# Routing and experts of a two-layer MoE block interleaved, with expert weights split ahead of time into a scratch in HBM

## The chip, the cores and the metric

The kernel runs on one core of one Trainium2 chip. The metric is device time in microseconds (us), from start to end of one execution. Everything is fp32 data; most matmuls are done as three products of a rounded "hi" part and a remaining "lo" part, so that the result keeps more than the precision of one product.

Five engines work in parallel, each on its own in-order stream, and meet by semaphores: PE (TensorE, matmuls), DVE (VectorE), ACT (ScalarE), POOL (GpSimd) and SP (SyncE, which here only issues DMAs). DMAs can be issued by SP, ACT and POOL.

## The reference

```python
# 1. gated linear attention, B=4, H=8, S=768, D=48
for t in range(S):
    state = f[:, :, t, :, None] * state + outer(k[t], v[t])
    y[t] = q[t] @ state
x = y as (3072 tokens, 384)
# 2. an MLP
h = x @ w_in                     # 384 -> 2048
x = maximum(0.01 * h, h) @ w_out # 2048 -> 384
# 3. a mixture of 8 experts, each with exactly 3072 / 8 = 384 tokens
logits = x @ w_gate
for idx in argsort(-logits.flatten()):       # greedy over all (token, expert) pairs
    tok, e = idx // 8, idx % 8
    if assigned[tok] < 0 and counts[e] < 384:
        assigned[tok] = e; counts[e] += 1
for e in range(8):
    out[assigned == e] = maximum(x[assigned == e] @ w1[e], 0) @ w2[e]   # 384 -> 1024 -> 384
```

## The kernel before

**Attention and MLP.** The four batches are pipelined: `both(eng, body)` runs `body(None, 0)` (attention of batch 0 alone), three rounds of `body(i, i + 1)` (MLP of batch i beside attention of batch i + 1), and `body(3, None)` (MLP alone). Every engine walks the same list, `schedule(mlp, att)`: 32 slots, each with one `up` (nine matmuls of 128x384 into `ps_h`) and one `down` (nine into `ps_acc`, for the `up` of three slots earlier, `LAG = 3`), and from slot 4 on one step of attention. Between `up` and `down` ACT scales (`leak`, L674), DVE takes the maximum (`leaky`, L836), ACT rounds (`round_g`, L683) and DVE forms the rest (`g_rest`, L843). There are two `ps_h` banks: the `up` of slot j needs the `leaky` of slot j - 2.

SP issues the loads of q, k, f and v for each pair of heads (`load_gates`, L377, and `load`, L391 and L396). It issues nothing else in this stage, so it stands well ahead of the other engines and waits there only for a buffer to come free.

**Routing.** The greedy assignment is done in seven phases, a loop on PE and DVE. A phase finds, for every token, its best open expert (`choose`), then in five rounds narrows down the value at which the first expert fills up: DVE compares 24 tiles of tokens with 32 thresholds (`compare`, L907), PE counts by 24 small matmuls (L1215), DVE and PE pick the interval (L970, L1219, L977). Then the tokens above it are taken, and the full expert is closed. Only when all seven phases and the last step are done does DVE turn the assignment into one list of token numbers, `perm`.

**Experts.** Then `expert_turns` runs experts 0 to 7 in order. Each is 24 + 24 units of three 128x384 matmuls. SP loads the raw weights of the next expert in four pieces of 768 KB (L415), ACT rounds them to `w_hi` (L726), POOL subtracts to get `w_lo` (L522). POOL gathers the expert's tokens by an indirect DMA (L529), PE turns them (`turn_rows`, L1250), and POOL scatters the results to `out` (L541).

Of the kernel before, what the change touches and what calls it, by code (L numbers as in the profile page):

```python
# [30 lines left out]
P = 128  # L31
# [26 lines left out]
PHASE_LINKS = 18  # L58


def gated_attention_two_mlps(nc, qkf, v, w_in, w_out, w_gate, w1, w2, out):
    x2_rows = nc.dram_tensor("x2_rows", (TOKENS, DM), F32, kind="Internal").ap()

    ctx = ExitStack()
    with ctx:
# [7 lines left out]
        w_hi = sb("w_hi", [P, 2, FF * KT], F32R)  # L73
        w_lo = sb("w_lo", [P, 2, FF * KT], F32R)
        w_raw = sb("w_raw", [P, 2, WCH])
        qk = sb("qk", [P, 2, 3, SEQ])
# [21 lines left out]
        x2_out = spare[:, KT * BLK:KT * BLK + ST * DM].rearrange("p (s d) -> p s d", s=ST)  # L98
        gate_w = sb("gate_w", [P, KT, EXPERTS])
# [9 lines left out]
        def carver(whole):  # L109
# [3 lines left out]
            def carve(*shape, dt=F32):  # L113
                n = int(np.prod(shape)) * (2 if dt == BF16 else 4) // 4
                got = whole[:, at[0]:at[0] + n]
# [13 lines left out]
        column = carve(P, dt=BF16)  # L129
        prefer = carve(EXPERTS, TT)  # L130
        slot0 = carve(EXPERTS, TT)
        tile_start = carve(TT)
        row = carve(1)
        earlier = carve(P, dt=BF16)
        ones = carve(P, dt=BF16)
        minus_earlier = carve(P, dt=BF16)
        minus_ones = carve(P, dt=BF16)

        carve = carver(xT[:].rearrange("p k t -> p (k t)"))
        magnitude, chosen, upto = (carve(EXPERTS, TT) for _ in range(3))  # L140

        prefer_open, taken, sure, above_low, maybe, fits = (carve(EXPERTS, TT, dt=BF16) for _ in range(6))
# [7 lines left out]
        open_, penalty = carve(EXPERTS), carve(EXPERTS)  # L150
        slot, slot_row, slot_tile = carve(TT), carve(TT), carve(TT)
        slot_int, slot_bits, slot_tile_bits = (carve(TT, dt=I32) for _ in range(3))

        carve = carver(log_f[:])
        above = carve(TT, WAYS, dt=BF16)
        counted = carve(EXPERTS, TT, dt=BF16)
        row_sure, row_maybe, filled, is_full = (carve(EXPERTS, dt=BF16) for _ in range(4))
        flag = carve(2, dt=BF16)
        restart_tile = carve(EXPERTS, TT, dt=BF16)
        carve = carver(y_pair[:].rearrange("p b n -> p (b n)"))  # L160
        row_hot = carve(TT, P, dt=BF16)
        carve = carver(qk[:].rearrange("p b a n -> p (b a n)"))
        tile_hot = carve(TT, TT, dt=BF16)
        tile_hot_start = carve(TT, TT, dt=BF16)
        tile_hot_row = carve(TT, TT, dt=BF16)
# [57 lines left out]
        y_rows_free = sem("y_rows_free")  # L223
        x2_stored = [sem(f"x2_stored{i}") for i in range(ST)]

        route_consts = sem("route_consts")
        most_local = sem("most_local")
        most_ready = sem("most_ready")
        routed = sem("routed")
        best_ready = sem("best_ready")  # L230
# [4 lines left out]
        keyed_ready = sem("keyed_ready")  # L235
        chosen_ready = sem("chosen_ready")
        sure_ready = sem("sure_ready")
        above_low_ready = sem("above_low_ready")
        penalized = sem("penalized")
        open_ready = sem("open_ready")  # L240
        row_sums_ready = sem("row_sums_ready")
        row_bases_done = sem("row_bases_done")
        slot_row_ready = sem("slot_row_ready")
        tile_hot_ready = sem("tile_hot_ready")
        hot_ready = sem("hot_ready")
        perm_done = sem("perm_done")
        perm_ready = sem("perm_ready")
        ewraw_in = [sem(f"ewraw_in{i}") for i in range(2)]
        ew_hi_done = sem("ew_hi_done")
        ew_lo_done = sem("ew_lo_done")  # L250
# [7 lines left out]
        edown_done = sem("edown_done")  # L258
        y_rows_ready = sem("y_rows_ready")
# [78 lines left out]
        def weight_piece(n, half):  # L338

            if half == 0:  # L340
                return (lambda w: w[:, 0, :].rearrange("p (k f) -> p k f", k=KT)[:, :, n * 512:(n + 1) * 512],
                        w_in.rearrange("(k p) f -> p k f", p=P)[:, :, n * 512:(n + 1) * 512], KT)
# [11 lines left out]
        def expert_turns(eng, turn):  # L354


            with eng.Fori(0, EXPERTS // 2 - 1) as i:
                for q in range(2):
                    turn(i * 2 + q, q, True, i)
# [958 lines left out]
```

## Time and profile before

| what | value |
|---|---|
| three runs | 1054.19, 1056.42, 1056.67 us; median 1056.42 |
| the profiled execution: span, first to last instruction | 1052.9 us |
| its PE, DVE, ACT, POOL busy | 843.3, 516.1, 352.8, 228.9 us |
| mean granted TensorE clock | 0.882 of full speed |
| DMA | 70.16 MB |

The whole execution of a run is the span and a few microseconds around it; the median of the runs is 3.5 us above this span. By stages: attention alone from 0 to about 104 us, three rounds of MLP beside attention to about 544, MLP alone to 656, routing to 817, experts to the end. A "busy" share says how long an engine had an instruction in work, not that it could not have done more.

### The profile page before, as it was taken

The page shows a single profiled execution, that of the slowest core. Times are in us where ns is not written, and L with a number is a line of the kernel's source. Part 1 is how long each engine was busy: PE and PEld are TensorE (multiplying, and loading weights), DVE is VectorE, ACT ScalarE, POOL GpSimd, SP SyncE. Part 2 cuts the span into 40 slices and gives each one's busy share as a digit, 9 for nine tenths or more (in the row PEclk, how much of TensorE's full clock was granted, in tenths as well). Part 3 has the DMA queues.
Part 4 walks back from the last instruction along what each step waited for, and adds up shares of the span by engine and source line. Part 5 has one row for each costly group of instructions (what it writes and reads, how often), then busy time and mean ns, then how long its engine had stood idle before and what let it go on. Part 6 is the DMA issues. An engine that isn't in the chain of part 4 may idle for free.

```text
span 1052.9 us, 16482 instructions
## 1 busy us (share of the span) xinstructions
PE 843.3 (80%) x5665; PEld 813.5 (77%) x5665; DVE 516.1 (49%) x1166; ACT 352.8 (34%) x737; POOL 228.9 (22%) x154
## 2 busy tenths in 40 slices
PE   2547999997999998999999998122322699999995
PEld 2446899997999997999999998122212699999994
DVE  7774755543655434656433333787788222222220
ACT  3233645433545334444323322200000244444431
POOL 7930000000000000000010000400000467777741
PEclk9678999998999998999999999555555799999998
DMA  8544223321023321122000000310000245555520
GB/s 214 142 89 93 42 45 58 79 47 36 13 45 65 77 41 36 42 40 37 25 30 1 1 23 23 122 58 0 0 0 1 75 136 164 164 164 164 165 83 23
DMA packets 53082, 70.16 MB, mean 67 GB/s; under 512 B 28752, under 2 KB 37712, under 8 KB 53008
## 3 DMA queue, kind: packets, MB, share of 16 engines
q1 hardware_dynamic: 44432, 44.06, 17.8%
q0 software_dynamic: 6208, 20.45, 5.9%
q10 hardware_dynamic: 2368, 4.72, 2.2%
q8 instruction: 39, 0.64, 0.3%
q14 instruction: 35, 0.29, 0.1%
HBM read 55.06 MB, written 9.44 MB: 61 GB/s over the span
## 4 chain that ended last, share of the span: by engine, by line
PE 72%; DVE 16%; issue 7%; ACT 2%; DMA 1%; POOL 1%; DVEq 0%; ACTq 0%; POOLq 0%
PE ps_h L1148 9%; PE ps_acc L1148 9%; PE ps_h L1150 9%; PE ps_h L1149 9%; PE ps_acc L1149 9%; PE ps_acc L1150 9%; PE ps_s L1100 4%; PE ps_y L1110 4%; PE ps_s L1215 3%; DVE log_f L907 2%; DVE cum L780 2%; PE ps_y L1115 1%; PE ps_k L1084 1%; DVE rel L786 1%; PE ps_h L1183 1%
## 5 line engine op out<-in xcount | busy, mean ns | idle before, releaser
L1148 PE MATMUL ps_h<-x_hi,w_hi 128*128 128x384 f32 x576 | 207.8, 361 | 11.1 <-issue 8.3
L1150 PE MATMUL ps_h<-x_hi,w_lo 128*128 128x384 f32 x576 | 198.2, 344 | 0.0
L1149 PE MATMUL ps_h<-x_lo,w_hi 128*128 128x384 f32 x576 | 198.2, 344 | 0.0
L836 DVE TENSOR_TENSOR g_full<-ps_h,g_full 128x384 f32<-128x384 f32 x128 | 71.3, 557 | 205.3 <-ACT g_full L674 205.1
L470 POOL DMA_DIRECT2D x_rows<-w_raw x24 | 13.1, 545 | 576.5 <-DVE logits L852 574.2
L1148 PE MATMUL ps_acc<-g_hi,w_hi 128*128 128x384 f32 x384 | 131.0, 341 | 0.0
L1149 PE MATMUL ps_acc<-g_lo,w_hi 128*128 128x384 f32 x384 | 130.0, 339 | 0.0
L1150 PE MATMUL ps_acc<-g_hi,w_lo 128*128 128x384 f32 x384 | 129.8, 338 | 0.0
L522 POOL TENSOR_TENSOR w_lo<-w_raw,w_hi 128x1536 fp32r<-128x1536 f32 x32 | 112.0, 3510 | 45.5 <-ACT w_hi L726 38.2
L1148 PEld LDWEIGHTS ps_h<-x_hi,w_hi 128*128 128x128 f32 x576 | 111.1, 193 | 13.4 <-issue 10.2
L674 ACT ACTIVATE g_full<-ps_h 128x384 f32<-128x384 f32 x128 | 62.5, 489 | 169.1 <-PE ps_h L1150 165.5
L1149 PEld LDWEIGHTS ps_h<-x_lo,w_hi 128*128 128x128 f32 x576 | 111.2, 193 | 0.0
L1150 PEld LDWEIGHTS ps_h<-x_hi,w_lo 128*128 128x128 f32 x576 | 110.8, 192 | 0.0
L1051 DVE SCALAR_TENSOR_TENSOR g_lo<-ps_h,g_hi 128x384 fp32r<-128x384 f32 x64 | 35.6, 557 | 124.8 <-ACT g_hi L740 124.8
L1215 PE MATMUL ps_s<-log_f 128*32 128x8 bf16 x840 | 28.9, 176 | 73.3 <-DVE log_f L931 39.0
L1215 PEld LDWEIGHTS ps_s<-log_f 128*32 128x32 bf16 x840 | 25.5, 103 | 76.3 <-DVE log_f L907 76.3
L616 ACT ACTIVATE y_pair<-ps_y 96x128 f32<-96x128 f32 x96 | 26.2, 273 | 161.0 <-PE ps_y L1115 136.7
L1148 PEld LDWEIGHTS ps_acc<-g_hi,w_hi 128*128 128x128 f32 x384 | 72.1, 188 | 0.0
L1149 PEld LDWEIGHTS ps_acc<-g_lo,w_hi 128*128 128x128 f32 x384 | 72.1, 188 | 0.0
L1150 PEld LDWEIGHTS ps_acc<-g_hi,w_lo 128*128 128x128 f32 x384 | 72.0, 188 | 0.0
L843 DVE TENSOR_TENSOR g_lo<-g_full,g_hi 128x384 fp32r<-128x384 f32 x128 | 70.4, 550 | 0.5
L1100 PE MATMUL ps_s<-q_apart,qk 112*128 112x256 f32 x192 | 66.5, 431 | 4.6 <-DVE scores L824 3.4
(165 smaller groups left out, 1484.9 us busy)
## 6 DMA issues: line engine op xcount, KB each, us to landing
w_raw<-w SPq DMA_DIRECT2D x32, 768.0 KB, 4.4
qk<-qkf SPq DMA_DIRECT2D x32, 288.0 KB, 5.3
qk<-qkf SPq DMA_DIRECT2D x32, 144.0 KB, 5.0
vals<-v SPq DMA_DIRECT2D x32, 144.0 KB, 6.7
x_rows<-w_raw POOLq DMA_DIRECT2D x24, 192.0 KB, 2.2
w_raw<-w_in POOLq DMA_DIRECT2D x4, 768.0 KB, 7.1
w_raw<-w_out POOLq DMA_DIRECT2D x4, 768.0 KB, 5.2
xT<-y_pair ACTq DMA_DIRECT2D x8, 192.0 KB, 5.9
```

The source lines that it names most:

```text
L522: nc.gpsimd.tensor_tensor(place(w_lo, q), w_raw[:, n % 2].rearrange("p (k f) -> p k f", k=tiles), place(w_hi, q).bitcast(F32), ALU.subtrac ...
L616: nc.scalar.activation(y_pair[0:2 * HD, hp % 2, c * P:(c + 1) * P], ps_y[0:2 * HD, 0:P], ACT.Copy).then_inc(y_copied, 1)
L674: nc.scalar.activation(g_full[:, j % 2, :], ps_h[j % 2][:, 0:BLK], ACT.Copy, scale=0.01)\
L836: nc.vector.tensor_tensor(g_full[:, j % 2, :], ps_h[j % 2][:, 0:BLK], g_full[:, j % 2, :], ALU.max).then_inc(g_ready, 1)
L843: nc.vector.tensor_tensor(g_lo[:, b, :], g_full[:, j % 2, :], g_hi[:, b, :].bitcast(F32), ALU.subtract).then_inc(g_lo_ready, 1)
L1051: nc.vector.scalar_tensor_tensor(out=g_lo[:, f % GB, :], in0=ps_h[f % 2][:, 0:CAP], scalar=0.0, in1=g_hi[:, f % GB, :].bitcast(F32), op0=A ...
L1100: nc.tensor.matmul(ps_s[:, 0:2 * P], qk[0:HP, hp % 2, 1, chunk], q_apart[:, :, chunk], start=True, stop=True).then_inc(scores_done, 1)
L1110: last = nc.tensor.matmul(y, vals[:, hp % 2, c, h * HD:h * HD + 2 * HD], scores[:, before % 2, h], start=h == 0, stop=c == 0 and h == 1)
L1148: nc.tensor.matmul(to, a_hi, b_hi, start=start, stop=False)
L1149: nc.tensor.matmul(to, a_hi, b_lo, start=False, stop=False)
L1150: last = nc.tensor.matmul(to, a_lo, b_hi, start=False, stop=stop)
L1215: last = nc.tensor.matmul(ps_s[0:WAYS, 0:EXPERTS], above[:, g, :], counted[:, :, g], start=g == 0, stop=g == TT - 1)
```

## The change

1. **Weights of the experts.** In each of the 32 slots of a round with an MLP, one more item, `prep`, stands behind `up`: SP loads a chunk of 128x384 of `w1` or `w2` into `e_raw` (192 KB), ACT rounds it to `e_hi` (`prep_hi`), DVE subtracts (`prep_lo`, in place), and SP stores both to the scratch `ready_weights` in HBM. Four rounds of 32 chunks are all eight experts. There are two `e_raw` buffers, and `store_prep` issues the load of chunk n + 1 behind the two stores of chunk n.
2. **Routing beside experts.** After each phase the expert that has just filled up is picked (`pick`, with its number in `weight_index`), its list of 384 tokens is formed (`place`, `gather_lists`, `list_tokens`), and it runs next. `expert_order()` merges the phases into the units of the experts by a table of gaps: phase 0 and, up to unit 64, the first part of phase 1 stand ahead of the first expert; a phase then takes 47 units and an expert 48.
3. **Fetch.** POOL fetches the split weights of the picked expert by four indirect DMAs (1.5 MB each), two ahead of the gather of the tokens and two behind. ACT's rounding and POOL's subtraction in the expert stage are gone. POOL's `partition_all_reduce` ahead of phase 0 becomes two small matmuls.

```diff
+        ready_weights = [nc.dram_tensor(f"ready_weights{n}", (EXPERTS * P, 2 * WCH), F32, kind="Internal").ap()
+                     for n in range(4)]
...
                     yield "up", h, j
+                    yield "prep", slot
...
+        def route_order():
+            at = 0
+            for p in range(EXPERTS - 1):
+                for gap, step in ((2, "choose"), (5, "count0"), (2, "ways0"), (3, "count1"), (2, "ways1"),
+                                  (3, "count2"), (2, "ways2"), (3, "count3"), (2, "ways3"), (3, "count4"),
+                                  (2, "ways4"), (4, "rank"), (3, "fill"), (3, "base"), (6, "spot"), (2, "spread")):
+                    at += gap
...
+            def store_prep(mb, n, last):
+                b = n % 2
+                _, _, to = prep_piece(mb, n)
+                sp.wait_ge(prep_hi_done, mb * 2 * FT + n + 1)
+                sp.sem_inc(prep_seen, 1)
+                sp.dma_start(to[0], e_hi[:, b, :]).then_inc(prep_hi_stored[b], 16)
+                sp.wait_ge(prep_lo_done, mb * 2 * FT + n + 1)
+                sp.sem_inc(prep_seen, 1)
+                sp.dma_start(to[1], e_raw[:, b, :]).then_inc(prep_lo_stored[b], 16)
+                if 1 <= n < 2 * FT - 1:
+                    prep_landed(mb, n - 1)
+                    load_prep(mb, n + 1)
...
                     elif what == "load":
                         load(ab, *a)
+                    elif what == "prep":
+                        store_prep(mb, a[0], ab is None)
...
+            def prep_hi(mb, n):
+                act.wait_ge(e_raw_in[n % 2], 16 * (mb * FT + n // 2 + 1))
+                nc.scalar.activation(e_hi[:, n % 2, :].bitcast(F32R), e_raw[:, n % 2, :], ACT.Copy)\
+                    .then_inc(prep_hi_done, 1)
...
+            def prep_lo(mb, n):
+                dve.wait_ge(prep_hi_done, mb * 2 * FT + n + 1)
+                nc.vector.tensor_tensor(e_raw[:, n % 2, :].bitcast(F32R), e_raw[:, n % 2, :], e_hi[:, n % 2, :],
+                                        ALU.subtract).then_inc(prep_lo_done, 1)
...
+            def load_expert(e, n):
+                q = e % 2
+                nc.gpsimd.indirect_dma_start(
+                    out=w[:, q, n].rearrange("p h n -> p (h n)").bitcast(F32), out_offset=None,
+                    in_=ready_weights[n][:, :],
+                    in_offset=bass.IndirectOffsetOnAxis(ap=weight_index[:, e:e + 1], axis=0)).then_inc(ew_in[q][n], 16)
```

**SP's stream at the head of a round of MLP beside attention.** Before, the round begins with the loads of f (48x768), of q and k (48x1536) and of v (128x6x48) for the first pair of heads:

```order
L334 ISA
L377 ISA [waits gates_zeroed0,exp_done]
L377 DMA qk<-qkf 48x768
L377 ISA
L377 DMA qk<-qkf 48x768
L265 REGISTER_ALU
L391 REGISTER_ALU [waits y_done,zeroed0]
L391 DMA qk<-qkf 48x1536
```

Now the stores of the split chunk 0 stand ahead of them, and these wait for ACT and DVE of slot 0 of the same round:

```order
L350 ISA
L483 ISA [waits prep_hi_done]
L483 DMA ready_weights<-w_raw 128x384
L486 ISA [waits prep_lo_done]
L486 DMA ready_weights<-e_raw 128x384
L280 ISA
L447 ISA [waits gates_zeroed0,exp_done]
L447 DMA qk<-qkf 48x768
L447 ISA
L447 DMA qk<-qkf 48x768
L280 REGISTER_ALU
L461 REGISTER_ALU [waits y_done,zeroed0]
```

The loads of the first pairs are no longer free to be issued during the round before.

**SP's stream in the slots of such a round** (there was nothing at this place before; `e_raw<-w` is the load of a chunk, `w_raw` holds `e_hi`):

```order
L486 DMA ready_weights<-e_raw 128x384 [waits prep_lo_done]
L470 ISA [waits prep_hi_stored1,prep_lo_stored1]
L470 DMA e_raw<-w 128x384
L481 REGISTER_ALU
L483 DMA ready_weights<-w_raw 128x384 [waits prep_hi_done]
L486 DMA ready_weights<-e_raw 128x384 [waits prep_lo_done]
```

The load of the next chunk is issued behind the store that waits for this chunk's `prep_lo`.

**DVE's stream in an expert beside a phase.** Before, nothing but `g_lo` and `x_lo` stood in an expert. Now the end of `fill`, all of `base` and the start of `spot` (from `pick` to `gather_lists`) stand between the `g_lo` that PE waits for:

```order
L1073 SCALAR_TENSOR_TENSOR qk<-vals,qk 128x24 [waits routed]
L1123 SCALAR_TENSOR_TENSOR g_lo<-ps_h,g_hi 128x384 [waits eg_hi_ready]
L1080 TENSOR_TENSOR qk<-qk,ps_k 128x24 [waits slot_base_done,reach_ready]
L1081 TENSOR_TENSOR qk<-qk 128x24 [waits routed]
L1082 TENSOR_SCALAR qk<-qk 128x24 [waits routed]
L1083 TENSOR_SCALAR qk<-qk 128x24 [waits routed]
L1084 TENSOR_SCALAR qk<-qk 128x24
L1085 TENSOR_TENSOR qk<-vals,qk 128x24x12 [waits routed]
L1087 TENSOR_TENSOR qk<-qk,vals 128x24x12 [waits routed]
L1088 TENSOR_SCALAR qk<-qk,vals 128x24x12 [waits routed]
L1089 TENSOR_TENSOR qk<-vals,qk 128x768
L1123 SCALAR_TENSOR_TENSOR g_lo<-ps_h,g_hi 128x384 [waits eg_hi_ready]
```

Nine operations on the lists stand between one `g_lo` and the next.

## Rows read from the trace of the kernel before

**Rows 1.** The head of the profile's page

```profile
span 1052.9 us, 16482 instructions
```

**Rows 2.** Windows by stage: start:end, length, busy us of each engine, clock, DMA

```profile
core 0: us, PE busy (x) PEld busy (x) DVE busy (x) ACT busy (x) POOL busy (x), PEclk, DMA share, GB/s
60.00:75.00 15.00, 10.18 (x46) 8.82 (x47) 8.45 (x15) 5.07 (x13) 2.62 (x1) 0.65 0.15 34
549.00:645.00 96.00, 96.00 (x555) 95.89 (x555) 33.78 (x69) 29.78 (x67) 3.25 (x12) 1.00 0.02 7
690.00:823.00 133.00, 35.00 (x820) 28.07 (x820) 102.43 (x364) 0.00 (x0) 5.65 (x5) 0.50 0.02 5
827.00:1010.00 183.00, 182.48 (x1047) 181.73 (x1048) 42.24 (x78) 82.38 (x123) 129.56 (x63) 0.99 0.48 151
```

**Rows 3.** Timeline of the MLP alone: start us, us, engine, line, operation

```profile
549.56 0.49 ACT L674 ACTIVATE g_full<-ps_h 128x384 f32<-128x384 f32 x1 [1.53 <-PE ps_h L1150]
550.09 0.56 DVE L836 TENSOR_TENSOR g_full<-ps_h,g_full 128x384 f32<-128x384 f32 x1 [1.46 <-ACT g_full L674]
...
641.58 0.49 ACT L674 ACTIVATE g_full<-ps_h 128x384 f32<-128x384 f32 x1 [2.28 <-PE ps_h L1150]
...
644.76 0.49 ACT L674 ACTIVATE g_full<-ps_h 128x384 f32<-128x384 f32 x1 [2.27 <-PE ps_h L1150]
```

**Rows 4.** Timeline, ACT: first and last slot of the first round beside attention

```profile
104.35 0.49 ACT L674 ACTIVATE g_full<-ps_h 128x384 f32<-128x384 f32 x1 [2.22 <-PE ps_h L1150]
...
235.61 0.49 ACT L674 ACTIVATE g_full<-ps_h 128x384 f32<-128x384 f32 x1 [2.27 <-PE ps_h L1150]
```

**Rows 5.** DMA issues: tiles, issuer, count, KB each, median us to landing

```profile
w_raw<-w SPq DMA_DIRECT2D x32, 768.0 KB, 4.4
...
qk<-qkf SPq DMA_DIRECT2D x32, 144.0 KB, 5.0
...
x_rows<-w_raw POOLq DMA_DIRECT2D x24, 192.0 KB, 2.2
...
gate_w<-w_gate SPq DMA_DIRECT2D x1, 12.0 KB, 1.8
```

**Rows 6.** Timeline, SP: the loads of one pair of heads

```profile
201.31 0.83 SPq L391 DMA_DIRECT2D qk<-qkf  x2
...
204.00 1.26 SPq L377 DMA_DIRECT2D qk<-qkf  x2
```

**Rows 7.** Window over the landing of these loads

```profile
202.00:210.00 8.00, 8.00 (x53) 7.84 (x52) 3.61 (x9) 2.23 (x6) 0.00 (x0) 1.00 1.06 192
```

**Rows 8.** Timeline of routing: its start, one phase, one count on PE

```profile
655.75 0.36 DVE L936 SCALAR_TENSOR_TENSOR xT<-logits 128x192 f32<-128x192 f32 x1
...
664.11 0.62 DVE L914 TENSOR_REDUCE xT<-logits 128x24 f32<-128x192 f32 x1 [0.20 <-DVE xT L950]
...
694.04 0.62 DVE L914 TENSOR_REDUCE xT<-logits 128x24 f32<-128x192 f32 x1 [0.41 <-DVE xT L1008]
...
711.19 0.17 DVE L1004 TENSOR_SCALAR xT<-ps_y 128x8 f32<-128x8 f32 x1
...
712.61 0.62 DVE L914 TENSOR_REDUCE xT<-logits 128x24 f32<-128x192 f32 x1 [0.39 <-DVE xT L1008]
```

**Rows 9.** Timeline, PE: the count of one round of a phase

```profile
717.72 0.82 PE L1215 MATMUL ps_s<-log_f 128*32 128x8 bf16 x24 [0.94 <-DVE log_f L907]
```

**Rows 10.** The chain that ended last: the first expert's start

```profile
820.99 3.04 DMA xT<-x_rows,perm
824.08 0.91 PE ps_s L1250 x3
...
827.52 0.68 PE ps_h L1148
```

**Rows 11.** Timeline, PE: the same turn of rows in two following experts

```profile
840.59 0.49 PE L1250 MATMUL ps_s<-ident,xT 128*128 128x128 f32 x3
...
867.00 0.49 PE L1250 MATMUL ps_s<-ident,xT 128*128 128x128 f32 x3
```

More of the change, by code:

```diff
@@ L258, in gated_attention_two_mlps @@
         edown_done = sem("edown_done")
+        y_rows_free = sem("y_rows_free")
         y_rows_ready = sem("y_rows_ready")
@@ new lines, in take @@
+            def take(p):
+                dve.wait_ge(row_bases_done, p + 1)
+                link(stt(out=fits, in0=upto, scalar=-(CAP + 0.5), in1=by_tile(ps_k[:, 16:24]),
+                         op0=ALU.add, op1=ALU.is_le))
+                link(tt(fits, fits, maybe, ALU.mult))
+                link(tt(taken, fits, sure, ALU.add))
+                whole_sum(filled, taken).then_inc(filled_ready, 1)
+                link(stt(out=logits[:], in0=taken, scalar=HUGE, in1=logits[:], op0=ALU.mult, op1=ALU.add))
@@ L1057, in _ @@
-            for k in range(KT):
-                rows_rest(0, 0, k)
-            expert_turns(dve, turn)
+            for what, *a in expert_order():
+                if what == "route":
+                    step, p, n = a
+                    if step == "choose":
+                        choose(p)
+                    elif step == "count":
+                        flag_full(p, n)
+                    elif step == "ways":
+                        narrow(p, n)
+                    elif step == "rank":
+                        take(p)
+                    elif step in ("fill", "last"):
+                        pick(p)
+                    elif step == "base":
+                        place(p)
+                    elif step == "spot":
+                        gather_lists(p)
+                    elif step == "spread":
+                        list_tokens(p)
+                elif what == "rows_rest":
+                    e, k = a
+                    rows_rest(e, e % 2, k)
+                elif what == "rest":
+                    g_expert_rest(*a)
@@ L1239, in _, with count_above @@
-            last.then_inc(perm_done, 1)
-            def turn_rows(e, q, k, earlier_users):
+            def count_above(p, n):
+                rnd = p * ROUNDS + n
+                if n == 0:
+                    pe.wait_ge(chosen_ready, p + 1)
+                for g in range(TT):
+                    for m, part in enumerate(PARTS):
+                        if g == part.start:
+                            pe.wait_ge(above_ready, rnd * len(PARTS) + m + 1)
+                    last = nc.tensor.matmul(ps_k[0:WAYS, 0:EXPERTS], above[:, g, :], counted[:, :, g],
+                                            start=g == 0, stop=g == TT - 1)
+                last.then_inc(counts_done, 1)
@@ new lines, in fills, with slot_base, token_lists @@
+            def fills(p):
+                pe.wait_ge(filled_ready, p + 1)
+                nc.tensor.matmul(ps_k[:, 24:32], ones, filled, start=True, stop=True).then_inc(fills_done, 1)
+            def slot_base(p):
+                pe.wait_ge(reach_ready, p + 1)
+                nc.tensor.matmul(ps_k[:, 32:33], earlier, reach[:, TT - 1:TT], start=True, stop=True)\
+                    .then_inc(slot_base_done, 1)
+            def token_lists(p):
+                pe.wait_ge(hots_ready, p + 1)
+                for g in range(TT):
+                    last = nc.tensor.matmul(ps_k[0:WIDE, 40:40 + 2 * SPOTS], wide_hot[:, g, :], spots[:, g, :],
+                                            start=g == 0, stop=g == TT - 1)
+                last.then_inc(narrow_done, 1)
```

684 lines of the change are left out of this document (367 added, 317 removed).

## The prediction

> **What bounds the kernel now.** I read the windows by stage first. In the MLP alone PE is busy for 96.00 of 96.00 us, in the experts for 182.48 of 183.00, both at full clock; in routing for 35 of 133 us at the clock's lower level (0.50, 1.2 GHz), while DVE is busy for 102.43 [rows 2]. So PE bounds everything but routing, and routing is a dialogue of DVE and PE in which no large matmul runs. A phase takes 18.57 us (694.04 to 712.61) [rows 8]. Routing and experts together take 397.2 us, from 655.75 [rows 8] to the end of the span at 1052.9 [rows 1]. An expert takes 26.41 us (840.59 to 867.00) [rows 11], 48 units of three matmuls. A slot of the MLP alone takes 3.18 us, and slots 1 to 31 take 95.2 us (549.56 to 644.76) [rows 3]. The 31 intervals of a round beside attention take 131.3 us (104.35 to 235.61) [rows 4], 4.23 each.
>
> **First part: routing beside experts, a gain.** I lay out the new way from 655.75 to the end.
> - *Prelude.* It took 8.4 us (655.75 to 664.11) [rows 8], most of it in waiting for POOL's reduce over partitions. With two small matmuls in its place I count 3.1 us.
> - *To the first expert.* In the steady phase, choose to the full counts takes 17.2 us (694.04 to 711.19) [rows 8]. `pick`, `place` and the lists add about 16 short DVE operations and the one-hots, which I put at 6.5 us: the list of tokens is there at 23.7. The part of phase 1 up to unit 64 (choose, three counts) stands next in PE's order, about 10 us; the gather of the tokens (three issues, then 3.04 us to land [rows 10]) and the first two weight pieces run beside it. From landed rows to the first `ps_h` it is 3.4 us (824.08 to 827.52) [rows 10]. Together 38 us.
> - *An expert beside a phase.* PE: 26.4 us, and six sets of 24 small matmuls (0.82 us a set [rows 9], of which about 0.65 keep PE from the next matmul) with some 25 changes between kinds of matmul, together 5.5 us: about 32. DVE: 18.57 us of a phase [rows 8], 6.1 more of new work, 11 `g_lo` and `x_lo` of 0.56 [rows 3]: 30.9 if none of the dialogue's waits is filled. Neither alone is over 32. But both streams are in a fixed order: `place` and its neighbours keep DVE for 3.5 us where PE has six units (3.2 us), `choose` with the end of the lists for 5 where PE has seven (3.7) and needs `g_lo` twice in between, and each round's compare takes 1.6 for three units of 1.6. I add 4 us of PE waiting. 36 us per expert; the bounds are 32 (no waiting) and 41 (each such place paid in full).
> - *Sum.* 342 units of phases less the 64 ahead are 278, or 5.8 experts at 36; the other 2.2 run at 26.4. The start and end of the stage beyond eight such experts are 225.4 - 211.3 = 14.1 us (from 827.52 [rows 10] to 1052.9). So 3.1 + 38 + 208.8 + 58.1 + 14.1 = 322 us in place of 397: **-75 us**, bounds -52 (41 us per expert) and -98 (32).
> - *The fetch* moves 6.3 MB of split weights and 1.2 MB of rows per expert. The stage now moves 151 GB/s with the DMA engines 0.48 busy [rows 2], so 315 GB/s if they were full: 24 us per expert, under the 36. Two pieces go ahead of the tokens, 10 us and 2 of latency; about 21 units and a dozen small steps lie between `pick` and `turn_rows`, 14 us. That is just hidden, and I cost it at nothing.
>
> **Second part: the preparation of the weights, a loss.** `prep` puts 128 chunks into slots that PE fills. Its ACT and DVE time (0.49 and 0.56 us each [rows 3]) finds room: in the MLP alone DVE is busy for 34 of 96 us. What counts is the loop it closes. The load of chunk n + 1 is issued only behind the store of chunk n's `lo`, and ACT, in order, stands at `prep_hi` of chunk n + 1 until it has landed, with `leak` of the next slot behind it; PE can be two slots ahead of that and then waits. So a slot cannot be shorter than this round trip, C:
> - ACT rounds and DVE starts: 0.53 us (549.56 to 550.09 [rows 3]); DVE subtracts: 0.56;
> - SP issues the `lo` store: 0.42 (half of a pair's 0.83 [rows 6]), with semaphores and address registers about 0.2 more, then issues the load;
> - its landing, L. No row shows a 192 KB load on SP alone. 12 KB took 1.8 us and 768 KB took 4.4; a 192 KB store 2.2 [rows 5]. Between the first two a straight line gives 2.4, and part of the `lo` store just ahead in the queue makes it 2.6. The lower bound is 2.2; the upper is 5.0, the 144 KB load that stood behind others [rows 5]. I take the near rows, 2.6.
>
> C = 0.53 + 0.56 + 0.42 + 0.25 + 2.6 = 4.4 us, 3.9 with the low L, 5.0 if L is 3.2.
> - *MLP alone:* the first two chunks are there ahead; 30 slots go from 3.18 to 4.4: **+37 us** (+22 to +55).
> - *Three rounds beside attention:* at 4.23 us per interval the loop alone costs little. The head costs more. The loads of q, k, f and v for two pairs used to be issued in the round before; now they stand behind the first `prep` stores of this round, and the load of chunk 2 behind them all, on the same queue. One pair's loads keep the DMA engines full from 202 to 210 us, busy share 1.06 [rows 7], after an issue of 4 us that began at 201.31 [rows 6]; less the latency I count 7 us. Two pairs are 14 us from about 3.5 us into the round, then two stores: chunk 2 lands at 19.4 us. After it come 29 intervals at 4.4, and two more pair loads in mid-round delay a chunk by 2.3 us each: 19.4 + 127.6 + 4.6 = 151.6 us in place of 131.3. **+20 us each, +61 in all**. With C at 3.9 and the head at 16 PE binds again behind the head, and a round costs +12; with C at 5.0, +38.
> - *Clock:* during the head PE is idle, and some matmuls behind it will run at the lower level, as all of routing does (0.50 [rows 2]), and take twice as long. I put +5 us on it for three heads, an estimate without a row of its own.
>
> **Sum.** 1052.9 - 75 + 37 + 61 + 5 = 1081 us of span; with the 3.5 us by which the median of the runs is above this span, **1085 us**. The forecast is a kernel slower by some 29 us.
>
> **Rivals.**
> 1. *The loop is hidden: faster.* If the load lands in under about 1.6 us, or the ring takes the load ahead of the queued stores and pair loads, C falls to the slot's 3.18, the last stage costs nothing, and only some 10 us of waiting for f and q remain per head. Then 1056 - 75 + 30 = 1011 us. It decides at C near 3.8 with a head of 9 us. For it: PE keeps two slots in hand. Against it: the one 192 KB row took 2.2 us to land [rows 5], and the sum of the rest is 1.8. A gain also comes if both bounds meet, -98 and +63. Chance 0.24.
> 2. *The experts wait for their fetch.* POOL now issues seven indirect DMAs for an expert, and DVE is at work on the lists beside it. If the tokens land 4 to 6 us late for each of seven experts: +35, 1120 us. For it: the slack is 2 us by my count. Against: the DMA engines are full for only two thirds of an expert. The stage now says little, since DVE is busy in it for only 42 of 183 us [rows 2]. The Trainium skill ("SBUF — State Buffer", Who interferes with whom) says that DVE in its two-port modes locks GpSimd out of the port it writes DMA descriptors through, and that DMAs issued by SP or ACT are immune; it speaks against moving the fetch from SP to POOL. No row here has POOL issuing beside a busy DVE. Chance 0.12.
> 3. *The clock falls in the last stage.* With C at 4.4 PE is busy for 72% of a slot. In the prologue a stretch with PE busy for 10.18 of 15 us had a mean clock of 0.65 [rows 2]. At 0.65 the 18 matmuls take 4.9 us, and a slot with them: +15, and at the full lower level, 5.8, +42; so 1100 to 1127, say 1110. The Trainium skill ("TensorE: Matmul & The Clock Gate", HAM oscillation — how this bites in real kernels) describes the same: bursts of matmuls between waits for a DMA run slow every time. Against it: a wait of 1.2 us is short beside those of the prologue. Chance 0.12.
> 4. *A longer loop.* L at 3.2 us, from 512-byte rows of `w1` and the store ahead: +18 in the last stage, +54 in the rounds: 1150 us. Chance 0.10.
>
> **How the numbers follow.** The forecast has 0.42, with a range of its own from 1060 to 1110. Rivals 2 to 4 make 0.34, all slower, rival 1 0.24. Measurement tells 0.3% (3 us) from no change. Faster: 0.26, of them 0.24 from rival 1; the same: 0.03, from the overlap of the bounds; slower: 0.71. The range for 8 in 10 leaves out the lower part of rival 1 and the upper part of rival 4: 1012 to 1145.
>
> **What the profile after will show.** If I am right: `leak` of the MLP alone comes every 4.4 us in place of 3.18, with ACT's `prep_hi` waiting for the DMA of `e_raw`; the first slots of a round beside attention take 35 us or more to slot 6 in place of 18; the first expert starts some 41 us after the last logits; six experts take about 36 us each and the last two 26.4. The prediction is wrong if the slots keep 3.18 us (then rival 1), if an expert beside a phase takes 31 or 41 us, or if `turn_rows` waits for the gathered rows (rival 2).

## The result, and the profile after

The changed kernel takes 1152.19 us (median of 4 runs, 1151.73 to 1155.2), the kernel before 1055.41: a ratio of 1.0934, 95% interval 1.0903 to 1.0965. It is slower by 97 us; I had said 29, and the range ended at 1145. The profiled execution of after has a span of 1150.3 us. All differences below are between profiled executions unless a median is named.

The page's head and the chain that ended last:

```profile
span 1150.3 us, 18015 instructions
...
PE 34%; DVE 22%; DMA 19%; issue 10%; ACT 6%; SPq 6%; another core or an unknown queue 1%; ACTq 0%; POOL 0%; DVEq 0%
```

DMA has 19% of the chain, nearly all of it loads of `e_raw`. I mark slots by the start of ACT's `leak` (`g_full<-ps_h`), as in [rows 3, 4]. "Beside attention" stands for the rounds in which MLP and attention share the engines. The parts of the span that changed:

| part | before | after | difference | forecast |
|---|---|---|---|---|
| three rounds beside attention, first slot to first slot | 149.0, 149.0, 145.3 | 183.6, 184.6, 177.6 | +102.6 | +61 and +5 |
| MLP alone, slots 0 to 31 | 97.2 | 131.4 | +34.2 | +37 |
| last logits to the end | 397.2 | 359.5 | -38 | -75 |

What is left, the attention ahead of the first slot, differs by less than 2 us.

**MLP alone.** Timeline of after, the steady state; SPq is SP's queue of issues, the bracket names the idle time ahead and its releaser:

```profile
701.56 0.34 SPq L470 DMA_DIRECT2D e_raw<-w  x1
703.93 0.53 ACT L778 ACTIVATE w_raw<-e_raw 128x384 fp32r<-128x384 f32 x1 [2.77 <-DMA e_raw<-w]
704.36 0.47 ACT L764 ACTIVATE g_full<-ps_h 128x384 f32<-128x384 f32 x1
704.49 0.56 DVE L936 TENSOR_TENSOR e_raw<-e_raw,w_raw 128x384 fp32r<-128x384 f32 x1 [2.60 <-ACT w_raw L778]
...
705.13 0.33 SPq L486 DMA_DIRECT2D ready_weights<-e_raw  x1
...
705.65 0.34 SPq L470 DMA_DIRECT2D e_raw<-w  x1
...
708.02 0.53 ACT L778 ACTIVATE w_raw<-e_raw 128x384 fp32r<-128x384 f32 x1 [2.78 <-DMA e_raw<-w]
```

This is the loop of the forecast, row by row: load issued to ACT 2.37, ACT to DVE 0.56, DVE to the store's issue 0.64, store to the next load's issue 0.52. Together 4.09 us a slot (I had 4.4), where TensorE alone needs 3.18 [rows 3].

**The head of a round.** SP's issues in the second round, whose slot 0 is at 286.25, and ACT's rows beside them:

```profile
287.41 0.37 SPq L483 DMA_DIRECT2D ready_weights<-w_raw  x1
288.04 0.36 SPq L486 DMA_DIRECT2D ready_weights<-e_raw  x1
288.76 0.90 SPq L447 DMA_DIRECT2D qk<-qkf  x2
290.01 0.84 SPq L461 DMA_DIRECT2D qk<-qkf  x2
291.03 1.36 SPq L466 DMA_DIRECT2D vals<-v  x2
...
296.96 0.91 SPq L447 DMA_DIRECT2D qk<-qkf  x2
298.22 0.38 SPq L483 DMA_DIRECT2D ready_weights<-w_raw  x1
298.86 1.20 SPq L486 DMA_DIRECT2D ready_weights<-e_raw  x1
300.52 0.99 SPq L470 DMA_DIRECT2D e_raw<-w  x1
```

```profile
306.27 0.52 ACT L778 ACTIVATE w_raw<-e_raw 128x384 fp32r<-128x384 f32 x1 [10.06 <-DMA e_raw<-w]
```

The loads of two pairs, and those of f for a third, stand between the stores of chunk 0 and those of chunk 1, and the load of chunk 2 comes behind all. It is issued 14.3 us into the round, and ACT gets it at 20.0 us (forecast 19.4), after a wait of 10.06.

**The experts.** `turn_rows` of the eight experts (PE L1370) begin at 831.92, 870.22, 911.37, 954.78, 996.71, 1038.31, 1077.39 and 1104.14: 38.3, 41.1, 43.4, 41.9, 41.6, 39.1 us beside a phase and 26.8 without one. Windows over four of the intervals, columns as in [rows 2]:

```profile
911.00:955.00 44.00, 40.82 (x334) 35.13 (x334) 25.75 (x88) 6.67 (x14) 10.06 (x10) 0.85 0.51 197
955.00:997.00 42.00, 37.22 (x311) 31.79 (x310) 26.28 (x90) 6.67 (x14) 9.87 (x10) 0.95 0.45 170
997.00:1038.00 41.00, 37.01 (x306) 31.74 (x304) 25.29 (x86) 6.66 (x14) 9.86 (x10) 0.91 0.54 208
...
1077.00:1104.00 27.00, 26.87 (x157) 26.45 (x156) 6.33 (x12) 6.67 (x14) 9.70 (x10) 1.00 0.80 324
```

The clock is below 1.00 beside phases and 1.00 in the last, which has none. Timeline of PE and windows of 2 us around one first count show when it falls:

```profile
904.57 0.33 PE L1263 MATMUL ps_h<-x_hi,w 128*128 128x384 f32 x1
906.19 0.80 PE L1327 MATMUL ps_k<-qk 128*32 128x8 bf16 x24 [1.29 <-DVE qk L1012]
...
909.17 0.18 PE L1333 MATMUL ps_k<-qk,vals 32*128 32x1 bf16 x1 [0.78 <-DVE qk L1019]
```

```profile
906.00:908.00 2.00, 1.81 (x30) 1.69 (x30) 0.90 (x3) 0.00 (x0) 1.54 (x2) 0.97 0.69 184
908.00:910.00 2.00, 1.22 (x5) 0.82 (x4) 0.74 (x4) 0.00 (x0) 0.00 (x0) 0.50 0.94 356
...
916.00:918.00 2.00, 2.00 (x9) 1.93 (x9) 1.65 (x6) 0.49 (x1) 0.00 (x0) 0.50 0.02 6
918.00:920.00 2.00, 2.00 (x32) 1.71 (x31) 0.50 (x2) 0.00 (x0) 0.00 (x0) 0.97 0.00 0
```

TensorE waits 1.29 us for `choose`, runs 24 small matmuls, and within 2 us the clock is at its lower level for some 10 us. Between 840 and 1104 us it falls five times (at about 884, 908, 949, 966 and 1031 us), each time within 3 us of the end of a wait of 0.8 to 1.6 us, or during one, and stays low for 3 to 10 us. The length of a wait does not tell it alone. After a longer one (DVE's `g_lo` stood behind `choose`; the row names no releaser) the clock stayed at 1.00:

```profile
990.76 0.45 PE L1261 MATMUL ps_h<-x_hi,w 128*128 128x384 f32 x1 [2.13 <-issue]
```

```profile
991.00:993.00 2.00, 2.00 (x31) 1.71 (x31) 0.00 (x0) 0.00 (x0) 0.95 (x1) 1.00 0.74 193
```

### The profile page after: what moved, and what is told of

It is laid out like the page before. It is cut to its first block, busy times and chain, and to the rows that moved or that the text cites. A ratio compares the mean times of both kernels' runs of the same rounds, so it can differ in the third digit from the quotient of the medians.

```text
span 1150.3 us, 18015 instructions
## 1 busy us (share of the span) xinstructions
PE 905.3 (79%) x5828; PEld 836.2 (73%) x5828; DVE 595.8 (52%) x1438; ACT 369.4 (32%) x833; POOL 146.9 (13%) x156
## 4 chain that ended last, share of the span: by engine, by line
PE 34%; DVE 22%; DMA 19%; issue 10%; ACT 6%; SPq 6%; another core or an unknown queue 1%; ACTq 0%; POOL 0%; DVEq 0%
DMA e_raw<-w 19%; PE ps_h L1261 5%; PE ps_acc L1261 4%; PE ps_h L1263 4%; PE ps_h L1262 4%; DVE e_raw L936 4%; PE ps_acc L1262 3%; PE ps_acc L1263 3%; ACT w_raw L778 3%; SPq L486 2%; PE ps_k L1327 2%; PE ps_s L1213 2%; DVE cum L868 2%; PE ps_y L1223 2%
## 5 line engine op out<-in xcount | busy, mean ns | idle before, releaser
L1261 PE MATMUL ps_h<-x_hi,w 128*128 128x384 f32 x576 | 219.6, 381 | 54.2 <-DVE g_full L924 30.9
L1262 PE MATMUL ps_h<-x_lo,w 128*128 128x384 f32 x576 | 202.8, 352 | 0.0
L1263 PE MATMUL ps_h<-x_hi,w 128*128 128x384 f32 x576 | 202.5, 351 | 0.0
L1261 PEld LDWEIGHTS ps_h<-x_hi,w 128*128 128x128 f32 x576 | 114.3, 198 | 68.1 <-DVE g_full L924 33.7
L936 DVE TENSOR_TENSOR e_raw<-e_raw,w_raw 128x384 fp32r<-128x384 f32 x128 | 71.1, 556 | 160.3 <-ACT w_raw L778 160.0
L1261 PE MATMUL ps_acc<-g_hi,w 128*128 128x384 f32 x384 | 135.0, 352 | 9.6 <-ACT w_raw L789 6.0
L1262 PE MATMUL ps_acc<-g_lo,w 128*128 128x384 f32 x384 | 132.9, 346 | 0.0
L1263 PE MATMUL ps_acc<-g_hi,w 128*128 128x384 f32 x384 | 132.3, 345 | 0.0
L1262 PEld LDWEIGHTS ps_h<-x_lo,w 128*128 128x128 f32 x576 | 114.9, 199 | 0.0
L1263 PEld LDWEIGHTS ps_h<-x_hi,w 128*128 128x128 f32 x576 | 114.4, 199 | 0.0
L1261 PEld LDWEIGHTS ps_acc<-g_hi,w 128*128 128x128 f32 x384 | 75.0, 195 | 11.4 <-issue 6.3
L1262 PEld LDWEIGHTS ps_acc<-g_lo,w 128*128 128x128 f32 x384 | 74.8, 195 | 0.0
L1263 PEld LDWEIGHTS ps_acc<-g_hi,w 128*128 128x128 f32 x384 | 74.3, 194 | 0.0
L1261 PE MATMUL ps_acc<-w,g_hi 128*128 128x384 f32 x192 | 74.1, 386 | 0.0
```

Source lines behind the costliest of these rows:

```text
L936: nc.vector.tensor_tensor(e_raw[:, n % 2, :].bitcast(F32R), e_raw[:, n % 2, :], e_hi[:, n % 2, :], ALU.subtract).then_inc(prep_lo_done, 1)
L1261: nc.tensor.matmul(to, a_hi, b_hi, start=start, stop=False)
L1262: nc.tensor.matmul(to, a_hi, b_lo, start=False, stop=False)
L1263: last = nc.tensor.matmul(to, a_lo, b_hi, start=False, stop=stop)
```

## The experiments

The theory: the round trip of a chunk and the order of SP's queue cost the 137 us of the rounds and the MLP alone, and the clock beside phases costs part of the experts' gain. The rivals: the added passes of ACT and DVE, or the added DMA traffic, cost it whatever the order.

**Load first.** `store_prep` waits for the buffer and issues the next load ahead of this chunk's stores:

```diff
             def store_prep(mb, n, last):
+                if 1 <= n < 2 * FT - 1:
+                    prep_landed(mb, n - 1)
+                    load_prep(mb, n + 1)
                 ...
                 sp.dma_start(to[1], e_raw[:, b, :]).then_inc(prep_lo_stored[b], 16)
-                if 1 <= n < 2 * FT - 1:
-                    prep_landed(mb, n - 1)
-                    load_prep(mb, n + 1)
```

> The load of the next chunk, and its waits for the two stores that free its buffer, stand ahead of the waits and stores of this chunk on SP's queue, so a chunk's load no longer hangs behind ScalarE's and VectorE's work on the chunk before. Theory (a slot can't be shorter than the round trip store - landing - load - landing - ScalarE - VectorE): the round trip now spans two slots, the MLP alone goes from 4.2 us a slot back to 3.2 to 3.4 (-27 to -34 us), the three rounds lose some 10 us each (the stall at the head of a round stays): 1080 to 1095 us. Rival (the added passes of ScalarE and VectorE in their in-order streams fill the slot by themselves): MLP alone stays over 4.0 us a slot and the time over 1135. Second rival (DMA traffic itself lengthens the MLP's transfers): the same.

1112.31 us, ratio 1.0554 (1.0500 to 1.0607); MLP alone 120.3 us, rounds 176.8, 175.5, 172.2. It took 11 us off the MLP alone, not 27 to 34, and 5 to 9 off a round; the expected 1080 to 1095 and the rivals' 1135 were both missed. The timeline shows what was left:

```profile
690.49 0.37 SPq L489 DMA_DIRECT2D ready_weights<-e_raw  x1
...
693.33 0.39 SPq L470 DMA_DIRECT2D e_raw<-w  x1
693.83 0.42 SPq L486 DMA_DIRECT2D ready_weights<-w_raw  x1
694.36 0.37 SPq L489 DMA_DIRECT2D ready_weights<-e_raw  x1
...
697.16 0.39 SPq L470 DMA_DIRECT2D e_raw<-w  x1
```

From one low store to the landing that SP waits for is 2.8 us, and the next load and the next two stores stand behind that wait: 3.9 us from store to store (690.49 to 694.36). The loop had only moved into SP's own queue.

**Chunks issued by GpSimd.** `load_prep`, `prep_landed` and `store_prep` go word for word from SP's stream to POOL's:

```diff
-                sp.dma_start(to[0], e_hi[:, b, :]).then_inc(prep_hi_stored[b], 16)
+                pool.dma_start(to[0], e_hi[:, b, :]).then_inc(prep_hi_stored[b], 16)
```

> All loads and stores of the split weights are issued by GpSimd's stream in place of SP's, in the same order among themselves. Theory (at a round's head the q, k and v loads stand on SP's queue behind the stores of the split chunks, whose waits hold them up): the stall of ScalarE on q, k at the head goes, each of the three rounds loses 12 to 18 us, and the slots with pair loads fall from 7.4 to about 5: 1095 to 1115 us; the MLP alone stays at 4.1 to 4.4 us a slot, since the round trip is as long as before (GpSimd's descriptor work may add to it). Rival (the round's added time is the round trip alone, wherever it is issued): rounds stay within 5 us of 184 and the time is over 1135.

1243.93 us, ratio 1.1812 (1.1760 to 1.1865): 92 us slower than the changed kernel. The head's first stall did go (slot 0 of the first round took 2.4 us in place of 7.7), but the rest lost more: MLP alone 167.3, rounds 206, 204, 194. A row pair says why:

```profile
766.65 0.75 POOL L563 DMA_DIRECT2D e_raw<-w  x1
...
769.62 0.52 ACT L778 ACTIVATE w_raw<-e_raw 128x384 fp32r<-128x384 f32 x1 [4.05 <-DMA e_raw<-w]
```

2.97 us from issue to ACT in place of 2.37, and the issues themselves take longer (0.75 us for this one, 0.34 on SP), so a slot of the MLP alone takes 5.3 us in the median. Beside a pair's loads, a chunk takes up to 8.0 us to land. The expected 1095 to 1115 was missed by far; the edit doesn't separate the order of the queue from the engine that issues. The Trainium skill ("DMA: Bandwidth & Descriptors", Issuing engine by pattern) gives simple loads and stores to Sync and calls that path generally faster; the traces agree, with these numbers.

**Both.**

> Both edits: the next load ahead of this chunk's waits, and all of them on GpSimd. If both theories hold and add up, rounds of 150 to 160 us and an MLP alone of 3.2 to 3.4 us a slot: 1025 to 1050 us, which is under the kernel before. If only the round trip matters: as the first of these runs, 1080 to 1095. If neither: over 1135.

1173.29 us, ratio 1.1144 (1.1104 to 1.1184); rounds 187.7, 188.4, 177.5, MLP alone 147.9. A miss by over 120 us. Slots of the MLP alone are mostly 4.4 to 4.6 us; I take it for the loop of the load-first kernel (3.7) at GpSimd's prices, which no run isolates.

**The splitting alone.** The kernel before, with `prep` added on all engines and nothing else. Its old experts don't use the result:

```diff
                     yield "up", h, j
+                    yield "prep", slot
```

> The kernel before with the splitting ahead alone: its loads, its two passes and its stores stand in the MLP slots as in the changed kernel, and the old routing and experts stay and don't use the result. If the change's parts add up: 1055 + 103 (rounds) + 34 (MLP alone) = 1192, within 1180 to 1200, and the routing and experts take 397 us from the last logits as before. If the parts interact (the new expert order makes up for some of it, or the new stage is slow because of the split's stores): under 1175.

1192.87 us, ratio 1.1329 (1.1282 to 1.1377). Rounds 185.7, 180.3, 180.2, MLP alone 131.2, as expected: the parts add up, +139 for the splitting and -41 for the rest. The chunks cost the same where the old experts run behind them.

**Three buffers.** `e_raw` gets a third buffer, loads run two chunks ahead, and ACT waits itself for the landing of the high store that frees `e_hi`. (`causal` and `pair_mask` become BF16 for the room.)

```diff
-        e_raw = sb("e_raw", [P, 2, BLK])
+        e_raw = sb("e_raw", [P, 3, BLK])
...
+                if n >= 1:
+                    prep_landed(mb, n - 1)
+                    if n < 30:
+                        load_prep(mb, n + 2)
```

> Three buffers for the raw chunks in place of two: a load is issued two slots ahead, ahead of this chunk's waits, once the low part's store of the chunk before has landed; ScalarE itself waits for the high part's store that frees its buffer. All still on SP. Theory (the round trip is what holds the slots; in the last run it spanned two slots, 7.46 us, so 3.73 each): over three slots it is 2.5 us a slot, under the 3.2 that TensorE needs, so the MLP alone goes to 3.2 to 3.4 us a slot (100 to 106 us in all, -15 to -20 against the load-first kernel's 120), and in the rounds only the head remains, shortened because chunk 2 is already there: 155 to 168 us each. Time 1050 to 1080. Rival (the added passes and the DMA traffic themselves slow the MLP): no better than the load-first kernel, 1105 to 1115.

1069.61 us, ratio 1.0137 (1.0093 to 1.0181); within the expected 1050 to 1080; rounds 165.2, 164.6, 162.1 as expected; MLP alone 116.1, not 100 to 106. The mid-round losses are gone, the 3.7 us slots are not.

**Early pair loads**, on the load-first kernel. SP's stream alone is reordered:

```diff
+                    if what == "attend" and a[0] == 19 and after is not None:
+                        load_gates(after, 0)
+                        load(after, 0)
...
+                        if a[0] == 29:
+                            next_pair_1()
```

> The load-first kernel with the attention's pair loads moved on SP's queue alone: those of pairs 0 and 1 of the next batch are issued in the round before, once their buffers are free, as in the kernel before; the others a slot later than they were, when what they wait for is done. Theory (at the head a slot is lost because f, q, k and v stand behind the last chunk's stores, and chunks 1 and 2 behind some 10 us of pair loads): slots 0 to 3 of a round fall from 28 us to 11 to 14, slots 11 to 18 lose most of their excess of 7 us, rounds 152 to 160 us; MLP alone stays at 120. Time 1050 to 1075. Rival (the head's stall comes from DMA traffic, not from order): rounds stay over 170 and the time over 1100.

1067.93 us, ratio 1.0154 (1.0106 to 1.0202), 44 us less than the same kernel without it. The time is within the expected 1050 to 1075. Slots 0 to 3 of the second round took 13.3 us in place of 25.8, the third round 149.7. The first two rounds stayed at 170.8 and 162.7, above what I expected. One chunk's load now stands behind pair 0's early loads (slot 25 took 9.1 and 8.0 us; 4.6 in the third round, which has none), and in the first round slot 0 takes 8.8 us: its first chunks were loaded behind pair loads, and their stores are issued only at 112.8 us.

**Both of these.**

> Three buffers and the early pair loads together. If the two causes are the whole of the prep's cost: rounds of 149 to 155 us, MLP alone 98 to 104 us, so only the experts' gain of 38 us remains: 1018 to 1035 us, faster than the kernel before by 2 to 3.5%. If something else in the added work costs time (port, passes, traffic): over 1045.

1040.43 us, ratio 0.9869 (0.9832 to 0.9907): 1.3% faster than the kernel before, though over the 1018 to 1035 expected. Rounds 164.6, 154.0, 149.7, MLP alone 115.1. Its timeline shows the remaining wait: SP issues the load, and only then the high store of a chunk that ACT had rounded a slot earlier; ACT waits for that store to land:

```profile
603.45 0.37 SPq L495 DMA_DIRECT2D ready_weights<-e_raw  x1
606.00 0.39 SPq L475 DMA_DIRECT2D e_raw<-w  x1
...
606.51 0.42 SPq L492 DMA_DIRECT2D ready_weights<-w_raw  x1
...
607.03 0.37 SPq L495 DMA_DIRECT2D ready_weights<-e_raw  x1
609.31 0.53 ACT L815 ACTIVATE w_raw<-e_raw 128x384 fp32r<-128x384 f32 x1 [2.51 <-DMA ready_weights<-w_raw]
```

The load itself waited for the low store of 603.45 to land. From low store to low store it is 3.58 us (603.45 to 607.03), and that loop on SP is the slot.

**Load behind the stores**, with the three buffers and early pair loads. The wait and the load go back to where the change had them, behind this chunk's two stores; the first three chunks are loaded at the start of the first attention.

```diff
-                if n >= 1:
-                    prep_landed(mb, n - 1)
...
                 sp.dma_start(to[1], e_raw[:, n % 3, :]).then_inc(prep_lo_stored[n % 3], 16)
+                if n >= 1:
+                    prep_landed(mb, n - 1)
```

> As the run with three buffers and early pair loads, which left the MLP alone at 3.7 us a slot: there SP waits for the last low part's store to land (2.8 us) before it issues the next chunk's stores (0.5 each), and that sum is the slot. Here the same wait and load stand behind this chunk's two stores, so the landing lies inside a slot; and the first three chunks are loaded at the start of the first attention, ahead of pair loads that held them up until 112 us. Theory: the MLP alone falls to 3.2 to 3.3 us a slot (97 to 102 us in all, from 115), the first round from 164 to 152 to 158: 1012 to 1028 us in all. Rival (3.7 us is what ScalarE's and VectorE's passes or the 150 GB/s of traffic allow): MLP alone stays over 110 and the time over 1032.

1030.42 us, ratio 0.9771 (0.9738 to 0.9805). MLP alone 98.0 us, rounds 153.8, 153.8, 149.2; the time is 2 us over the expected 1012 to 1028. The six executions range from 1023.8 to 1038.1, and the profiled one is the slowest of them. A window over the MLP alone:

```profile
580.00:640.00 60.00, 59.49 (x345) 58.52 (x344) 27.22 (x58) 23.93 (x56) 1.65 (x3) 1.00 0.57 185
```

PE is busy for 59.49 of 60 us at full clock with 185 GB/s beside it. All passes and all traffic are still there, so in the MLP alone neither rival costs more than 1 us (98.0 against 97.2). In the rounds beside attention they may: 4.8, 4.8 and 3.9 us more than in the kernel before are left. In the second round much of it sits in slots 6, 13 and 19 (0.5, 0.6 and 0.7 us more than before), and slots 6 and 13 are longer by the same amounts in load first and three buffers, whatever the order. So of the 137 us some 122 were order and buffers; the other 14 are the added work's own, and no run divides them between passes and traffic.

**Keep busy.** In phases 2 to 6 of the changed kernel, matmuls that nobody reads fill TensorE's waits:

```diff
+            def keep_busy(times):
+                for _ in range(times):
+                    nc.tensor.matmul(ps_acc[1][:, BLK:BLK + P], ident[:], ident[:], start=False, stop=False)
...
             def count_above(p, n):
+                if n == 0 and p > 1:
+                    keep_busy(5)
...
             def count_ways(p, n):
+                if n == 0 and p > 1:
+                    keep_busy(3)
```

> The changed kernel with small matmuls whose result nobody reads (ident by ident into unused columns of ps_acc): five ahead of the first count and three ahead of the first sum over ways of phases 2 to 6, where TensorE waits 0.8 to 1.4 us for VectorE and the granted clock then falls to half for some 9 us. Theory (the experts take 41 us in place of 36 largely since those waits bring the clock down): the mean clock from the second expert's start to the seventh's end rises from 0.92 to 0.97 or more and the experts from 41.5 to 38 to 40 us, -6 to -14 us in all: 1138 to 1146. Rival (the fall of the clock isn't tied to these waits, or the added matmuls cost what they save): 1150 to 1158.

1142.02 us, ratio 1.0840 (1.0790 to 1.0890), 10 us under the changed kernel. Intervals of the experts: 38.6, 37.5, 38.1, 44.3, 38.2, 37.8, in sum 11 less, with the clock at 1.00 in four of the six. Where it fell five times in the changed kernel, it now falls once. One of these:

```profile
870.00:907.00 37.00, 35.92 (x322) 31.64 (x320) 25.88 (x89) 6.66 (x14) 10.09 (x10) 1.00 0.53 204
```

The time is within the expected 1138 to 1146. The interval of 44.3 has a wait that the edit doesn't fill, and the clock falls right behind it, at 954.0. (A second one of 2.12 us, at 980, costs its own length and no clock.)

```profile
953.83 0.57 PE L1261 MATMUL ps_h<-x_hi,w 128*128 128x384 f32 x1 [1.57 <-DVE x_lo L1118]
```

**The same on the best kernel.**

> The same with the small matmuls ahead of the first count and the first sum over ways of phases 2 to 6, which took 10 us off the changed kernel. If that gain is one of the clock in the experts' stage alone, it comes again in full: 7 to 12 us under the run beside it, 1002 to 1020 us. If it was of the run's scatter, within 3 us of it.

1025.47 us, ratio 0.9743 (0.9715 to 0.9770), 5 us under the run beside it, whose interval (0.9738 to 0.9805) overlaps this one: between the two cases I had set (1002 to 1020, or within 3 us), and not resolved. In the profiled pair the six intervals sum to 240.5 against 250.0, but that pair is the fastest execution of this kernel beside the slowest of the other, so it decides nothing.

The slots of the second round, each from its `leak` to the next, in us:

```
slot                  0    1    2     3    4    5    11   12   17   18   19   round
before                2.3  1.6  4.5   2.9  2.1  5.0  4.6  4.3  4.7  4.3  5.4  149.0
after                 7.4  1.6  13.1  5.0  4.0  7.3  5.6  7.5  5.4  10.1 6.6  184.6
load first            7.4  1.6  12.5  4.3  4.0  5.1  4.6  7.2  4.7  8.4  6.4  175.5
three buffers         7.5  1.6  5.0   8.2  3.7  5.0  4.6  4.5  4.7  4.5  6.1  164.6
load behind stores    2.7  1.6  5.0   3.3  2.1  5.0  4.6  4.5  4.7  4.5  6.1  153.8
```

## Why the prediction was right or wrong

**The direction and the mechanism were right, terms were mis-sized.** The span was off by 69 us (1150 against 1081): 37 in the rounds and 37 in the routing and experts, less 3 in the MLP alone and 2 ahead of the first slot. Three terms, in fact: the slots of a round behind its head, the clock in the rounds, and the expert beside a phase.

**Right: the round trip.** C was 4.09 us in the MLP alone and 4.5 behind the head (306.27 to 310.79), against 4.4; the MLP alone lost 34 us against 37. That it is order and buffers, not work, is shown for the MLP alone: the same work in another order runs at 3.2 us a slot.

**Right: the head.** ACT had chunk 2 at 20.0 us against 19.4. Slots 0 to 4 of the second round lost 17.6 us. On the load-first kernel the early pair loads gave back 12.5 in slots 0 to 3. That it agrees to 0.6 us is in part luck: I had counted the bytes of two pairs, and the queue held the f loads of a third as well.

**Wrong: "After it come 29 intervals at 4.4, and two more pair loads in mid-round delay a chunk by 2.3 us each".** Slot 31 of the second round began 168.5 us after slot 0, where I had 151.6:

```profile
454.77 0.48 ACT L764 ACTIVATE g_full<-ps_h 128x384 f32<-128x384 f32 x1
```

Chunk 2 was there at 306.27; from there to 454.77 it is 148.5 us in place of 132. Two things are in it. In the second round the slots with pair loads lost 4.9 us (slots 11 to 13) and 8.0 (slots 17 to 20), 12.9 in place of 4.6. SP's queue is held for 2.4 us by the pair's four issues, and the chunk behind them lands late.

```profile
348.00 0.89 SPq L461 DMA_DIRECT2D qk<-qkf  x2
349.07 1.33 SPq L466 DMA_DIRECT2D vals<-v  x2
...
352.61 0.47 SPq L470 DMA_DIRECT2D e_raw<-w  x1
...
357.94 0.52 ACT L778 ACTIVATE w_raw<-e_raw 128x384 fp32r<-128x384 f32 x1 [2.98 <-DMA e_raw<-w]
```

ACT had that chunk 5.3 us after its issue in place of 2.4, and at the second pair 6.0 us (385.52 to 391.56). I had priced the delay in the queue and not the landing behind the pair's own bytes. The other 8 us: before, slots 3 to 30 already took 4.4 us on average, but from 2.1 to 5.8 each, so a loop of 4.4 adds to the short ones and the long ones give nothing back. Slots 3 and 4 lost 3.9 us and the others from 5 on 6.4, most of it in slots 5 and 30 (2.3 and 1.2). Load first brought those 6.4 to 1.1, so nearly all of them are the loop's. It isn't a simple floor, though: slots 10, 16, 28 and 29 stayed at 4.1, 4.1, 3.8 and 3.3 us. These shares are read from one trace. That the losses as a whole are the loop's and the queue's is shown by load behind the stores, which removed all but 4 to 5 us of each round.

**Wrong: "I put +5 us on it for three heads", the clock in the rounds.** The three rounds as one window each, in before, in after and with the load behind the stores:

```profile
104.35:547.54 443.19, 428.95 (x2623) 417.31 (x2622) 232.38 (x486) 189.85 (x445) 9.81 (x18) 0.98 0.23 46
102.68:648.48 545.80, 450.99 (x2624) 432.16 (x2623) 277.83 (x582) 235.88 (x540) 9.80 (x18) 0.93 0.52 144
107.11:563.88 456.77, 434.27 (x2624) 418.61 (x2623) 273.05 (x582) 231.70 (x540) 9.78 (x18) 0.97 0.59 169
```

With the same matmuls PE was busy for 22 us more, at a mean clock of 0.93 in place of 0.98. So of the 102.6 us some 22 are matmuls that ran slower and 81 are PE's idle time, for which I had 5 and 61. This is a second way to divide the same 102.6 us, not an addition to the slots above. With the waits gone, most of the 22 went too.

**Wrong: "36 us per expert".** It was 40.9 (245.5 for the six intervals with a phase), at the upper bound of 41 and what I had named as a sign of being wrong. Of it, 26.8 is the expert, as expected. PE was idle for 4.5 us of an interval on average, near the 4 that I had put on waiting. It was busy for 36.4 in place of "about 32". At full clock, without filler, its busy time was 33.7 to 35.2 us in other kernels (35.0 in three buffers, 919.28 to 956.61); so 2 to 3 us are small matmuls and changes between kinds of matmul beyond my 5.5, and the rest is the lower clock, a term that I had only for the rounds and as a rival only for the MLP alone. In keep busy the intervals at full clock took 37.5 to 38.2; filling some of the waits gave 1.8 us per expert back. The Trainium skill ("TensorE: Matmul & The Clock Gate", HAM oscillation — how this bites in real kernels) describes bursts between waits that run slow; I used it for the stage with DMA waits, where the clock stayed at 0.97, and not for the one with waits for VectorE, where it was 0.85 to 0.97.

Of the 37 us in this part the six intervals are 31. Another 4 are the start: the first `ps_h` of an expert came 45.2 us after 790.84, not 41.1.

```profile
790.84 0.36 DVE L1129 SCALAR_TENSOR_TENSOR qk<-logits 128x192 f32<-128x192 f32 x1
836.06 0.69 PE L1261 MATMUL ps_h<-x_hi,w 128*128 128x384 f32 x1 [1.17 <-DVE x_lo L1118]
```

**Slips in the sums.** The prelude took 3.5 us (3.1). The bound "-52 (41 us per expert)" is a slip: 5.8 experts at 41 us make 351 us in the sum, -46. The forecast with 41 us per expert is then 1110 us of span, still 40 short of the one measured.

**The rivals.** 1, the loop is hidden: false here, and true of the kernel with the load behind the stores. 2, experts wait for their fetch: false; from the second expert on, `turn_rows` follows the matmul ahead of it without a gap, and no wait of PE for weights is in the trace. 3, the clock in the MLP alone: false, 0.97. 4, a longer loop: its 1150 us is the span that came, by luck and not by its cause; L was 2.4 to 2.5, not 3.2.

**Left open.** Experts' intervals at full clock came out at 37.3 to 38.2 us in some runs and 39.1 to 39.4 in others that share the experts' code; both edits has one of each. In the fifth interval of three buffers (37.3) PE is busy for 35.0 us and idle for 2.3, in that of load behind the stores (39.3) busy for 35.2 and idle for 4.1. So the 2 us are waits, not work; what sets them isn't settled. Nor is it settled which wait brings the clock down: one of 2.1 us in the same place of an expert did so in load behind the stores (at 874), and not in the changed kernel (at 990).

## What to carry to other kernels

A prefetch with a buffer to spare is not yet ahead: what counts is the longest wait in the issuing queue, and a wait for a landing (2 to 3 us) must have a whole stage of other work behind it. Put unrelated loads that are needed later ahead of such a chain or after it where you can, not between, and count their bytes as delay of the next landing. Compare a loop's time with each slot and not only with the mean: the mean of uneven slots hides what the short ones lose. Where small dependent steps are woven into a dense stream, count what a wait of 1 us can cost in clock besides the wait itself; here filler in some of the waits gave back 10 us of 1152.

## What the runs showed of the hardware that I had not expected

- Waits of TensorE of 0.8 to 1.6 us, in a stream otherwise dense, were followed in five places of after within 3 us by the lower clock level for 3 to 10 us (908 to 918 is one of the longest). In other places waits of up to 2.1 us were not (990 in after). In the MLP alone, waits of 0.9 us in every slot of 4.1 left it at 0.97.
- At the lower level matmuls of 384 columns started 0.32 us apart (910.73, 911.05, 911.37 in after), at full clock 0.18 (869.87, 870.05): 1.8 times, not twice.
- 185 GB/s of loads and stores, the DMA engines 0.57 busy, cost a fully busy TensorE nothing: 3.18 us a slot (load behind the stores, 580 to 640), as with 7 GB/s [rows 2, 3].
- The same 192 KB load took 2.5 us to land from SP (after) and 2.8 from GpSimd (chunks issued by GpSimd) in the median. The longest were 6.9 us and 8.0; on SP in load first it was 8.0 too, so the longest don't tell the issuers apart.
- From the last slot to the end, profiled executions ranged from 357 to 375 us among kernels with the same experts, in part by the clock (0.81 to 1.00 in an interval) and in part by waits; a change of 5 us there can't be read from one trace. Of load behind the stores, the fastest execution (1023.8 us) had a mean clock of 0.934 and the slowest (1038.1) 0.912.
